# Order of the expert loads: the rows of the next group ahead of a group's weights, and two weight blocks instead of four ahead of the first gather

## The chip, the cores and the metric

One core of a Trainium2 chip. The metric is device microseconds (us) of one execution, median over runs; lower is better. Engines are TensorE (PE, with PEld for its weight loads), VectorE (DVE), ScalarE (ACT), GpSimd (POOL) and SyncE (SP), each of which takes its instructions in order; a wait on a semaphore holds back everything behind it on that engine.

## The reference

Three stages. First a gated linear attention over 4 batches, 8 heads, 768 positions and head width 48, with a complex decay:

```python
for t in range(S):
    new_re = ar * S_re - ai * S_im
    new_im = ar * S_im + ai * S_re
    S_re, S_im = (new_re + kv, new_im)
    y[:, :, t] = np.einsum('bhd,bhde->bhe', q[:, :, t], S_re)
```

Then a mixture of experts with one expert for each token (3072 tokens of width 384, 8 experts of inner width 1024), and last a dense gated layer of inner width 1536:

```python
e_idx = np.argmax(x @ w_gate + modality_bias[modality_id], axis=1)
for e in range(E):
    mask = e_idx == e
    h = np.maximum(x[mask] @ w1[e], 0.0)
    out[mask] = gate_w[mask, None] * (h @ w2[e])
...
g = x @ w_gate
return (silu(g) * (x @ w_val)) @ w_out
```

## The kernel before

The attention runs in chunks of 128 positions and ends with all 24 tiles of 128 rows scaled and stored to `x_scratch`. The router's result is turned into a sorted order of the tokens (`sorted_id`) and, for each group of 384 sorted rows, the number of its expert (`tab` row 0) and the row at which the group begins (`tab` row 1). There are 8 groups' worth of rows and at most 15 groups; here the expert stage runs 9 groups and loads weights for 10.

**The expert stage.** A group t has 8 steps, numbered w = 8t to 8t+7; one step takes 128 of the 1024 inner columns. "Block w" is that step's slice of both expert matrices: two DMAs of 192 KB, issued by SP on lines 724 and 727, into one of RAW = 6 raw buffers. ACT turns the block into the high part of a two-part product (line 1455, `expert_high`), DVE makes the low part (line 1167, `expert_low`, semaphore `s_wl`). Both run AHEAD = 2 steps in front: in step w, ACT does relu(w) and then `expert_high(w+2)`; DVE does `h_low(w)`, then `expert_low(w+2)`, and then, in three steps of each group, a part of the next group's transposed rows (`x_evac`, lines 1160 and 1162). PE does `up(w)` (line 1714, 9 matmuls, waits for `expert_low(w)`), `down(w-1)` (line 1727, 9 matmuls) and in the same three steps a transpose of the next group's rows (`xtr`, line 1701). The three steps are 4, 5, 6 of group 0 and 2, 3, 4 of each later group. In the first step of each group ACT also copies the last group's result out of PSUM (`y_out`, line 1482) when `down` of the last group's step 7 is done.

**The rows.** POOL gathers the first group's rows (three indirect DMAs, line 543, semaphores `s_xf`) straight into the row buffer `xg`. For each later group t it gathers three tiles into a single staging buffer (line 551), waits for them, and stores them in order to `xs_scratch` (line 559, semaphore `s_xs`, 16 more for each group). The gather for group t begins only when the store for group t-1 has landed. From group 3 on it also waits for a step of PE. SP then reads group t's rows from `xs_scratch` with one DMA of 576 KB (`load_rows(t)`, line 738), for which it waits until `s_xs` says that group t is stored (line 732). ACT issues the dense layer's weights in between (line 1465), two of 384 KB when the first rows are gathered, and then one in every third step.

**The order on SP before.** Blocks 0 to 3 go out at once; then SP waits for the first group's three gathers (line 746), and issues blocks 4 to 7, then waits for the store of the first group's rows and for the zeroed tail of `xs_scratch`, and issues `load_rows(1)`. In each later group t, blocks 8t to 8t+3 come first, then `load_rows(t+1)`, then blocks 8t+4 to 8t+7. Block w needs its raw buffer free, which is `s_wl` of at least w-5.

Of the kernel before, what the change touches and what calls it, by code (L numbers as in the profile page):

```python
# [5 lines left out]
def build(nc, q, k, v, a_re, a_im, modality_id, moe_w_gate, modality_bias, w1, w2,  # L6
# [20 lines left out]
    FC = FE // P  # L27
# [21 lines left out]
    MG = NG + NE - 1  # L49
    RAW = 6  # L50
    SLOTS = 4
    AHEAD = 2
# [17 lines left out]
    with ctx:  # L70
# [3 lines left out]
        def sem(name):  # L74
            return ctx.enter_context(nc.semaphore(name))
# [226 lines left out]
        s_zero = sem("xs_zeroed")  # L302
        s_xf = [sem(f"first_rows{i}_gathered") for i in range(TG)]
        s_xs0 = sem("first_rows_stored")
# [39 lines left out]

        X_AT = (2, 3, 4)
        X_AT_FIRST = (4, 5, 6)

        ROWS_FIRST = 4

        PRODUCTS = ((0, 1), (1, 0), (0, 0))  # L350

# [5 lines left out]
        def first_steps(t):  # L357
            return range(t * FC, (t + 1) * FC)
# [19 lines left out]
        def after(eng, x, count):  # L378

            if count > 0:  # L380
                eng.wait_ge(x, count)
# [194 lines left out]
        def _(sp):  # L576
# [141 lines left out]
            def load_weights(w, e):  # L718
                t, f = divmod(w, FC)

                if w >= RAW:
                    sp.wait_ge(s_wl, w - RAW + 1)
                at = w_raw[:, w % RAW]
                sp.dma_start(at[:, 0:KC * P].rearrange("p (k f) -> p k f", k=KC),
                             w1_v[:, ds(e, 1), :, f * P:(f + 1) * P].rearrange("p o k f -> p (o k) f")
                             ).then_inc(s_wr[w % RAW], 16)
                sp.dma_start(at[:, KC * P:PIECE],
                             w2_v[:, ds(e, 1), f, :].rearrange("p o d -> p (o d)")).then_inc(s_wr[w % RAW], 16)

            def load_rows(t):  # L730
                sp.wait_ge(s_tab, 1)
                sp.wait_ge(s_xs, 16 * min(t, NG - 1))
                first = sp.value_load(tab[0:1, 1, t:t + 1], min_val=0, max_val=TOK)

                if t >= 2:
                    sp.wait_ge(s_xTp, KC * (t - 1))
                    after(sp, s_xl[t % 2], 16 * ((t - 1) // 2))
                sp.dma_start(xg[:, t % 2], xs_dram[ds(first, GW), :].rearrange("(i p) d -> p i d", p=P)
                             ).then_inc(s_xl[t % 2], 16)

            def load_group(t):
                e = sp.value_load(tab[0:1, 0, t:t + 1], min_val=0, max_val=NE - 1)
                for w in first_steps(t):
                    if w == ROWS_FIRST:
                        for i in range(TG):
                            sp.wait_ge(s_xf[i], 16)
                    if t > 0 and w % FC == FC // 2 and t + 1 < MG:
                        load_rows(t + 1)
                    load_weights(w, e)
                if t == 0:  # L750
                    sp.wait_ge(s_xs0, 16)
                    sp.wait_ge(s_zero, 16)
                    load_rows(1)

            sp.wait_ge(s_te, 1)
            for t in range(NG + 1):
                load_group(t)
            total = sp.value_load(tab[0:1, 2, 0:1], min_val=NG, max_val=MG)
            more_groups(sp, total, NG + 1, NG, load_group)

            def load_group_yT(g):
# [1043 lines left out]
```

## Time and profile before

| | |
|---|---|
| median of 3 runs | 1021.33 us (1021.08 to 1025.95) |
| the profiled execution | 1021.33 us, span 1019.6 us |
| PE busy | 936.1 us (92%) |
| DVE, ACT, POOL busy | 579.2, 382.2, 175.6 us |
| mean granted TensorE clock | 0.975 |
| expert stage, first to last `up` or `down` | 301.5 to 546.5 us |

The span is the time from the first to the last instruction; 1.73 us lie around it. Times in the rows below count from the start of the span. A DMA's landing is counted from the start of its issue.

### The profile page before, as it was taken

Reading aid. Unit: us, or ns where it says so; the run is one execution under the profiler, and the core shown is the slowest. Engines: PE = TensorE matmul, PEld = TensorE weight load, DVE = VectorE, ACT = ScalarE, POOL = GpSimd, SP = SyncE. Lnnn points to the kernel's source line nnn. Section 1 sums busy time; section 2 is a strip of 40 time slices with the busy share of each in tenths; the row PEclk is TensorE's granted clock in tenths of the full one; section 3 lists DMA queues with packets and bytes.
Section 4 is the critical chain, followed back from the end, with each engine's and each line's share of the span. In section 5 each row is a group of like instructions: output and inputs, shape, how many; then the busy total and the mean of one; then the engine's idle time right before and its main releaser. Section 6 shows DMA issues by size and latency. Waiting matters only on the chain.

```text
span 1019.6 us, 15885 instructions
## 1 busy us (share of the span) xinstructions
PE 936.1 (92%) x6100; PEld 888.9 (87%) x6100; DVE 579.2 (57%) x993; ACT 382.2 (37%) x536; POOL 175.6 (17%) x198
## 2 busy tenths in 40 slices
PE   2688999999959999999999999999999999999994
PEld 0566878888839999999998999999999999999994
DVE  6978777755566666666555445544444444535432
ACT  7987878756434545444342110111101111011110
POOL 6234234531842211100000001010101000010101
PEclk9799999999959999999999999999999999999998
DMA  9998743420368987765454000000101000000000
GB/s 170 156 156 117 112 88 49 63 56 1 126 215 273 331 280 249 248 201 173 153 187 136 1 24 24 24 24 3 45 1 47 1 24 24 24 24 1 24 1 23
DMA packets 211487, 98.83 MB, mean 97 GB/s; under 512 B 150854, under 2 KB 206406, under 8 KB 211403
## 3 DMA queue, kind: packets, MB, share of 16 engines
q1 hardware_dynamic: 197994, 70.19, 30.3%
q0 software_dynamic: 4368, 14.75, 4.2%
q10 hardware_dynamic: 9040, 12.78, 3.9%
q8 instruction: 51, 0.84, 0.3%
q14 instruction: 34, 0.27, 0.1%
HBM read 77.58 MB, written 20.08 MB: 96 GB/s over the span
## 4 chain that ended last, share of the span: by engine, by line
PE 79%; ACT 5%; DVE 5%; issue 5%; DMA 2%; SPq 2%; POOL 1%; ACTq 0%; DVEq 0%; POOLq 0%
PE psum L1759 27%; PE psum L1771 15%; PE psum L1714 9%; PE psum L1727 9%; PE psum L1568 4%; PE psum L1577 3%; PE psum L1558 2%; PE psum L1613 2%; PE psum L1547 2%; PE psum L1594 2%; PE psum L1616 1%; SPq L587 1%; PE psum L1549 1%; PE psum L1701 1%; ACT group_work L1482 1%
## 5 line engine op out<-in xcount | busy, mean ns | idle before, releaser
L1759 PE MATMUL psum<-xT_parts,w_parts 128*128 128x384 f32 x1728 | 316.3, 335 | 2.3 <-DVE xT_parts L1210 2.3
L1759 PEld LDWEIGHTS psum<-xT_parts,w_parts 128*128 128x128 f32 x1728 | 302.3, 189 | 2.6 <-issue 2.6
L1218 DVE TENSOR_TENSOR group_work<-group_work,psum 128x384 f32<-128x384 f32 x96 | 53.2, 554 | 233.1 <-ACT group_work L1526 233.1
L1526 ACT ACTIVATE group_work<-psum 128x384 f32<-128x384 f32 x96 | 47.2, 492 | 355.3 <-PE psum L1759 355.3
L1771 PE MATMUL psum<-w_parts,act_parts 128*128 128x384 f32 x864 | 166.3, 335 | 5.7 <-DVE act_parts L1226 5.7
L1771 PEld LDWEIGHTS psum<-w_parts,act_parts 128*128 128x128 f32 x864 | 150.7, 188 | 8.4 <-DVE act_parts L1226 8.4
L1714 PE MATMUL psum<-xT_parts,expert_parts 128*128 128x384 f32 x648 | 129.3, 344 | 5.4 <-DVE expert_parts L1167 4.5
L1727 PE MATMUL psum<-act_parts,expert_parts 128*128 128x384 f32 x648 | 123.9, 335 | 0.4 <-DVE act_parts L1172 0.4
L1714 PEld LDWEIGHTS psum<-xT_parts,expert_parts 128*128 128x128 f32 x648 | 113.4, 191 | 8.4 <-DVE expert_parts L1167 6.7
L1727 PEld LDWEIGHTS psum<-act_parts,expert_parts 128*128 128x128 f32 x648 | 112.9, 188 | 1.1 <-DVE act_parts L1172 0.8
L569 POOL DMA_INDIRECT out<-group_work,sorted_id x24 | 23.6, 981 | 462.3 <-ACT group_work L1532 457.4
L1167 DVE TENSOR_TENSOR expert_parts<-group_work,expert_parts 128x768 fp32r<-128x768 f32 x74 | 70.9, 958 | 33.0 <-ACT expert_parts L1455 32.2
L1476 ACT ACTIVATE act_parts<-psum 128x384 fp32r<-128x384 f32 x72 | 35.3, 490 | 125.3 <-PE psum L1714 125.3
L1172 DVE SCALAR_TENSOR_TENSOR act_parts<-psum,act_parts 128x384 fp32r<-128x384 f32 x72 | 40.1, 557 | 57.9 <-ACT act_parts L1476 57.9
L1455 ACT ACTIVATE expert_parts<-group_work 128x768 fp32r<-128x768 f32 x74 | 62.2, 841 | 10.8 <-DMA group_work<-in_w 5.9
L1315 ACT ACTIVATE arena<-psum 128x1024 f32<-128x1024 f32 x48 | 49.2, 1024 | 37.3 <-PE psum L1568 37.3
L867 DVE TENSOR_TENSOR arena<-psum,causal 128x512 f32<-128x512 f32 x48 | 33.1, 690 | 46.7 <-PE psum L1577 46.4
L1568 PE MATMUL psum<-ident,arena 128*128 128x128 f32 x384 | 54.0, 285 | 5.7 <-DVE arena L861 4.1
L1568 PEld LDWEIGHTS psum<-ident,arena 128*128 128x128 f32 x384 | 42.7, 144 | 15.2 <-issue 10.4
L1226 DVE TENSOR_TENSOR act_parts<-group_work,act_parts 128x384 fp32r<-128x384 f32 x96 | 53.7, 559 | 3.3
L1219 DVE TENSOR_TENSOR group_work<-group_work,psum 128x384 f32<-128x384 f32 x96 | 53.1, 554 | 3.3
L1577 PE MATMUL psum<-arena 128*128 128x128 f32 x384 | 51.9, 279 | 0.0
(192 smaller groups left out, 1041.6 us busy)
## 6 DMA issues: line engine op xcount, KB each, us to landing
group_work<-in_w SPq DMA_DIRECT2D x160, 192.0 KB, 3.5
group_work<-xs_scratch SPq DMA_DIRECT2D x10, 576.0 KB, 4.7
yT_scratch<-group_work ACTq DMA_DIRECT2D x9, 576.0 KB, 4.4
arena<-in_q SPq DMA_DIRECT2D x24, 192.0 KB, 4.0
arena<-in_k SPq DMA_DIRECT2D x24, 192.0 KB, 4.2
arena<-in_v SPq DMA_DIRECT2D x24, 192.0 KB, 4.4
x_scratch<-x_all SPq DMA_DIRECT2D x24, 192.0 KB, 1.9
xs_scratch<-group_work POOLq DMA_DIRECT2D x8, 576.0 KB, 5.9
```

The costliest lines, as they stand in the source:

```text
L1167: nc.vector.tensor_tensor(low, w_raw[:, w % RAW], high.bitcast(F32), ALU.subtract).then_inc(s_wl, 1)
L1218: link(nc.vector.tensor_tensor(sig[:, w % 2, :], sig[:, w % 2, :], psum[:, w % 2, 0:GW], ALU.mult))
L1219: link(nc.vector.tensor_tensor(sig[:, w % 2, :], sig[:, w % 2, :], psum[:, 2 + w % 2, 0:GW], ALU.mult))
L1226: nc.vector.tensor_tensor(low, sig[:, w % 2], high.bitcast(F32), ALU.subtract).then_inc(s_act, 1)
L1315: nc.scalar.activation(qkT[:, u % 3], psum[:, 2:4, :], ACT.Copy).then_inc(c_tev, 1)
L1455: nc.scalar.activation(we_p[:, w % SLOTS, 0], w_raw[:, w % RAW], ACT.Copy).then_inc(s_wh, 1)
L1568: last = nc.tensor.transpose(psum[:, 2 + j, hh * P:(hh + 1) * P], qk_nat[:, n % 3, j, HG * g + hh, :], ident[:])
L1577: last = nc.tensor.matmul(psum[:, 4 + u % 2, at], qkT[:, u % 3, 1, at], qkT[:, u % 3, 0, at], start=True, stop=True)
L1714: last = nc.tensor.matmul(psum[:, w % 2, 0:GW], we_p[:, w % SLOTS, i, k * P:(k + 1) * P], x_p[:, j, t % 2, k, :], start=(k == n == 0), sto ...
L1727: last = nc.tensor.matmul(psum[:, 4 + k, 0:GW], we_p[:, w % SLOTS, i, at:at + P], act_p[:, j, w % 2], start=(f == n == 0), stop=(f == FC - ...
L1759: last = nc.tensor.matmul(psum[:, b, 0:GW], wt[:, i, k, f * P:(f + 1) * P], x_p[:, j, g % 2, k, :], start=(k == n == 0), stop=(k == KC - 1 ...
L1771: last = nc.tensor.matmul(psum[:, 4 + i, 0:DM], act_p[:, a, w % 2, i * P:(i + 1) * P], w_o_p[:, c, f, :], start=(f == n == 0), stop=(f == ...
```

## The change

The constant ROWS_FIRST goes away. SP now waits for the first group's gathers in front of block 2 instead of block 4. It issues `load_rows(1)`, with its waits, in front of block 6 instead of behind block 7. For each later group t, `load_rows(t+1)`, with its wait for the store of group t+1, stands in front of block 8t instead of block 8t+4. No instruction is added or removed on any engine, and no buffer changes.

```diff
-        ROWS_FIRST = 4
-
...
             def load_group(t):
                 e = sp.value_load(tab[0:1, 0, t:t + 1], min_val=0, max_val=NE - 1)
+                if t > 0 and t + 1 < MG:
+                    load_rows(t + 1)
                 for w in first_steps(t):
-                    if w == ROWS_FIRST:
+                    if w == AHEAD:
                         for i in range(TG):
                             sp.wait_ge(s_xf[i], 16)
-                    if t > 0 and w % FC == FC // 2 and t + 1 < MG:
-                        load_rows(t + 1)
+                    if w == RAW:
+                        sp.wait_ge(s_xs0, 16)
+                        sp.wait_ge(s_zero, 16)
+                        load_rows(1)
                     load_weights(w, e)
-                if t == 0:
-                    sp.wait_ge(s_xs0, 16)
-                    sp.wait_ge(s_zero, 16)
-                    load_rows(1)
```

## Rows read from the trace of the kernel before

**Rows 1.** The page: the chain that ended last, shares of the span by engine.
```profile
PE 79%; ACT 5%; DVE 5%; issue 5%; DMA 2%; SPq 2%; POOL 1%; ACTq 0%; DVEq 0%; POOLq 0%
```
**Rows 2.** The chain that ended last, from 300 to 337: start, us, what.
```profile
300.34 6.65 DMA group_work<-x_scratch,sorted_id
307.28 6.54 DMA xs_scratch<-group_work
314.63 4.37 DMA group_work<-xs_scratch
319.05 0.55 PE psum L1701 x3
...
322.75 0.33 PE psum L1701 x3
...
329.66 1.56 PE psum L1714 x9
331.22 1.57 PE psum L1727 x9
...
334.70 0.86 ACT expert_parts L1455
335.57 0.97 DVE expert_parts L1167
336.59 1.83 PE psum L1714 x9
```
**Rows 3.** SP's timeline: issues of blocks 2, 4, 8, of rows 2, of block 12.
```profile
290.91 0.40 SPq L724 DMA_DIRECT2D group_work<-in_w  x1
...
299.86 0.38 SPq L724 DMA_DIRECT2D group_work<-in_w  x1
...
315.78 0.39 SPq L724 DMA_DIRECT2D group_work<-in_w  x1
...
329.95 0.38 SPq L738 DMA_DIRECT2D group_work<-xs_scratch  x1
...
331.07 0.50 SPq L727 DMA_DIRECT2D group_work<-in_w  x1
```
**Rows 4.** SP's waits over the whole span: us in total, times, longest.
```profile
SPq L732 <- DMA xs_scratch<-group_work: 17.5, 3, 8.3
```
**Rows 5.** POOL's timeline: gathers and a store, idle time before them in brackets.
```profile
293.42 1.25 POOL L543 DMA_INDIRECT group_work<-x_scratch,sorted_id  x1 [3.06 <-DVE sorted_id L1152]
...
297.84 0.95 POOL L551 DMA_INDIRECT group_work<-x_scratch,sorted_id  x1 [0.30 <-issue]
...
324.08 0.80 POOL L559 DMA_DIRECT2D xs_scratch<-group_work  x1 [6.43 <-DMA group_work<-x_scratch,sorted_id]
...
329.43 0.98 POOL L551 DMA_INDIRECT group_work<-x_scratch,sorted_id  x1 [4.55 <-DMA xs_scratch<-group_work]
```
**Rows 6.** L727, block 4's second DMA, issued at 300.43: its landing.
```profile
DMA to landing us min/median/max: 6.4/6.4/6.4
```
**Rows 7.** L727, block 12's second DMA, issued at 331.07: its landing.
```profile
DMA to landing us min/median/max: 6.6/6.6/6.6
```
**Rows 8.** L559, all seven stores of sorted rows: their landing.
```profile
DMA to landing us min/median/max: 4.6/5.2/7.2
```
**Rows 9.** ACT and DVE timeline: parts of block 2, then ACT's part of block 8.
```profile
305.28 0.84 ACT L1455 ACTIVATE expert_parts<-group_work 128x768 fp32r<-128x768 f32 x1
...
306.15 0.96 DVE L1167 TENSOR_TENSOR expert_parts<-group_work,expert_parts 128x768 fp32r<-128x768 f32 x1 [0.18 <-ACT expert_parts L1455]
...
325.06 0.84 ACT L1455 ACTIVATE expert_parts<-group_work 128x768 fp32r<-128x768 f32 x1
```
**Rows 10.** Windows of 1 us: busy PE, PEld, DVE, ACT, POOL, clock, DMA share, GB/s.
```profile
547.00:548.00 1.00, 0.00 (x0) 0.00 (x0) 0.47 (x2) 0.62 (x1) 0.00 (x0) 1.00 0.61 171
...
549.00:550.00 1.00, 1.00 (x4) 1.00 (x5) 0.96 (x3) 0.00 (x0) 0.00 (x0) 0.50 1.02 361
...
552.00:553.00 1.00, 1.00 (x7) 1.00 (x7) 0.00 (x0) 0.48 (x1) 0.00 (x0) 1.00 0.00 0
```

## The prediction, made before the changed kernel ran

> **What bounds the kernel now.** I read the page first. Its chain that ended last is PE for 79% of the span, and waits for a DMA make up 2% [rows 1]. So the kernel is bound by TensorE, and an order of loads can only matter where PE has run out of weights or of rows. I then followed that chain in order of time through the start of the expert stage, since only there does it leave PE for transfers [rows 2]. The reader is to see this in it: the gathers for group 1 (until 306.99), the store of its sorted rows (307.28 until 313.82) and the read of those rows (314.63 until 319.00) stand one behind the other, and PE's first transpose of group 1 starts on that read's landing, at 319.05. From there on the chain is up and down, 1.56 us each, with one short detour over ACT and DVE at the group's first steps (334.70 to 336.59). SP's own timeline tells what was issued when [rows 3], SP's waits show that line 732, the wait for the stored rows, held the queue three times, 8.3 us at most [rows 4], and POOL's timeline shows when each sorted group was stored [rows 5]. The last view is that of the clock beside a short pause of PE [rows 10].
>
> The point to keep: line 732 costs nothing in the kernel before, although SP stands there for 8.3 us, because the blocks that PE needs meanwhile were issued ahead of it. Blocks 8 to 11 went out from 315.78 on [rows 3], and SP then waited for group 2's rows until 329.95. The change puts this same wait ahead of block 8.
>
> **Part 1: blocks 2 and 3 behind the first gathers.** Before, they are issued from 290.91 on [rows 3] and are on the DMA engines while POOL issues the first gathers. The first gather's issue lasts 1.25 us, one issued later into a quieter stretch 0.95 us [rows 5], so 0.3 us each for about two of them, and perhaps 0.1 us of the last landing: I take 0.7 us earlier for the landing of the last first gather. Bounds: 0, if the longer issue has another cause, and 0.9 if all three are 0.3 us shorter. Everything behind it starts that much earlier: PE's first transposes, the dense loads, SP's next issues.
>
> What it costs: block 2 now has the place that block 4 had, issued at 299.86, second half at 300.43, which landed after 6.4 us [rows 3, 6], so at 306.8; ACT took block 2 at 305.28 [rows 9]. Block 2 is thus 1.5 us late for ACT. Its low part on DVE would end at 308.7 in the old times instead of 307.1, and PE takes up(2) at about 308.5, behind down(0). The cover is 1.3 us, so some 0.3 us are lost. Block 3 behind it is wanted a step (3.1 us) later and has the cover. Both fall together with PE's wait for group 1's rows, which stands anyway until they land, so the 0.3 us vanishes there. Part 1 alone: 0.7 us won (0 to 0.9).
>
> **Part 2: rows 1 ahead of blocks 6 and 7.** The bytes in flight between 300 and 314 don't change: four blocks, 2 to 5 in place of 4 to 7. The store of group 1 still ends at 313.8 less 0.7, so rows 1 are issued and land as before, less 0.7. Block 6 now follows them. It had been in its buffer long before. Issued at about 314.4 and 315.0 (0.7 us earlier than the old times, and 0.5 to 1.1 us behind the rows), it lands after 6.4 to 6.6 us, if the two blocks' second halves that were issued beside the same kind of traffic are a guide [rows 6, 7], at about 321.5. ACT's high part takes 0.84, DVE's low part 0.96 [rows 9]. In DVE's queue the first part of group 1's transposed rows stands behind that low part, and PE's second transpose waits for it; it ran at 322.75 before [rows 2]. Now it runs at 321.5 + 0.84 + 0.96 + 1.1 (two DVE passes over the rows) = 324.4, against 322.05 with the 0.7 taken off: 2.4 us of waiting (0 if block 6 lands in 4 us). This counts only if block 8 is in time, because a later wait for a fixed landing swallows it.
>
> **Part 3: rows 2 ahead of block 8.** Here the terms of the sum are. Queued on SP behind the wait for group 2's store are blocks 8 to 13. On ACT, relu(7), two dense weight copies and block 9 stand behind block 8; on DVE, the last part of group 1's rows and h_low(7); PE then stands in front of up(8), since nothing ahead of it in its own queue is left after down(6).
>
> - The store of group 2 ended 0.3 us before POOL's next gather at 329.43, so at 329.1 [rows 5]. It moves by the 0.7 of part 1, and by up to 0.5 because blocks 10 and 11 are not in flight beside it (it took 5.1, the shortest of all seven 4.6 [rows 8]). I take 328.0; bounds 327.0 and 329.3.
> - SP's wait to its issue of rows 2: 329.95 - 329.1 = 0.8. Rows 2 go out at 328.8.
> - Block 8 is next. Block 12 had exactly this place before: rows 2, then block 12, beside the same gathers of group 3. Its second half was issued at 331.07 and landed after 6.6 us, at 337.7, which is 7.7 us after rows 2 were issued at 329.95 [rows 3, 7]. So block 8 lands at 336.5. Bounds: 6.4 and 8.7 us instead of 7.7.
> - High and low part: 0.86 + 0.97 with the gaps between, 1.9 in all [rows 2]. up(8) starts at 338.4. Before, it started at 329.66 [rows 2]. That is 8.7 us later, and PE stands idle for about 7 of them, from down(6)'s end at some 331.4.
> - The clock. After a pause of 2 us between the expert and the dense stage PE's granted clock fell to 0.50 (1.2 GHz) as work began again and was back at 1.00 three us later, [rows 10]. Three to three and a half us at half rate are 1.6 us lost. A longer pause should do at least this once: 1.6, bounds 0 and 3.2.
>
> What is late next: nothing for long. h_low(7) and the copy of group 0's result come late by the same amount and their own chain from down(7)'s end to up(10), 332.8 to 336.6 before, keeps its 3.8 us [rows 2]. Blocks 9 to 13 follow block 8 at once, since their buffers are free. Rows 3, 4 and on stand ahead of blocks 16, 24 and on, and are reached 4 blocks earlier than before. Group 3's store was issued at 339.5 and was the slowest of the seven, 7.2 us [rows 8]; it ended at 346.7, so block 16 would go out at some 347 and land at 355, and ACT wants it in step 14, 13 us after up(10), which is past 360. From group 4 on POOL's store is finished some 7 us before SP gets there. These moves are hidden, and would cost whole microseconds in each group if that distance were gone. Nothing waits later that could give the time back: PE is the bound to the end, and a late group stays late.
>
> **Sum:** 8.7 + 1.6 = 10.3 us, made against the profiled execution's own 1021.33 us, which is the median of the runs as well: 1031.6 us.
>
> One rule of the Trainium skill bears on the 328.0. Row: group 2's gathers, on POOL's queue, landed at 323.8, 0.3 us before the store's issue at 324.08 [rows 5], while SP's blocks 8 to 11 were queued from 315.78 on [rows 3]. The page DMA: Bandwidth & Descriptors, section Queues, rings and completion order, says that each DMA engine takes turns between the queues with work, a packet at a time. By that, blocks 10 and 11, last in SP's own queue, take nothing from the gathers while 8 and 9 are undrained, and the store begins where I have it; if all queued bytes shared equally, two blocks fewer of about eight would bring the gathers in some 1.5 us earlier, and the sum would be 8.8 us, 1030.1. No row before separates the two.
>
> The same page, section Rules for kernel authors, speaks against the change: issue a DMA early, wait for it late. Block 8 goes out 13 us later than before. By the rule the time is worse.
>
> **Rivals.**
>
> *A. Faster or level: less traffic brings the sorted rows in time.* The sort is a chain of gather, store, gather, store. Part 1 frees it of two blocks. For block 8 to be ready at 329.66 it must land at 327.7, rows 2 must be issued by 320.0, and group 2's store must have landed by 319.2, ten us earlier than it did. For it: in quiet stretches a store takes 4.6 [rows 8] instead of 6.5 [rows 2], and a group of gathers three issues of 0.95 with 0.3 between and some 3 us to land, about 5.6, instead of the 9.2 from 297.84 to 306.99 [rows 2, 5]; two of each from 297.8 give some 318.5. Against it: after 300 the same number of blocks and the same two dense loads are in flight as before, so the stretch isn't quiet; only 0.7 us is won at its head. If it came out so, only part 1 is left: 1020.6, or 1023.0 with block 6's wait. The point from which it decides is group 2's store landing before 320. For a gain of over 5 us no row offers a source.
>
> *B. Slower, but half as much.* Block 8 overtakes part of the rows' traffic, or the dense load that now is held back on ACT leaves room, and the clock stays up: 327.0 + 0.8 + 6.4 + 1.9 = 336.1, 6.4 us late, 1027.8.
>
> *C. Slower by more.* No gain from part 1 (329.3), block 8 lands after 8.7 us since six blocks are now issued in one burst, and two stretches at half clock: 329.3 + 0.8 + 8.7 + 1.9 - 329.7 = 11.0, plus 3.2, is 14.2: 1035.5.
>
> **Chances.** The sum within 2 us, 0.50; B and what lies between, 0.22; C and beyond, 0.14; A 0.10, and in it 0.03 for a gain over 0.5%; 0.04 for anything else that leaves it within 0.5%. 0.5% is 5.1 us, about what a measurement of this kernel can tell from no change. So faster 0.03, same 0.11, slower 0.86. The range that holds 8 in 10 leaves out A and the far end of C: 1027.0 to 1035.0.
>
> **What would show it.** In the profile after: the last first gather lands near 299.0; block 2's high part starts near 306 and up(2) is within 0.5 us of where it was; rows 1 land near 318.3; PE's second transpose of group 1 comes about 2 us late; group 2's store lands near 328, rows 2 are issued near 328.8, block 8 near 329.4, and PE stands idle from about 331 to 338 in front of line 1714, released by DVE's line 1167; the granted clock falls to 0.5 there; from step 10 on the distance to the kernel before stays near 10 us. SP's waits name line 732 for more than 17.5 us, and line 724 for less. The prediction is wrong if group 2's rows are stored before 320, if block 8 lands in less than 5 us, or if rows 3 and later hold SP long enough for a second wait of PE.

## The result, and the profile after

| | before | after |
|---|---|---|
| median of 7 runs | 1021.51 us (1021.08 to 1025.95) | 1031.44 us (1028.12 to 1036.35) |
| profiled execution, and its span | 1021.33, 1019.6 us | 1028.27, 1026.5 us |
| up(0) starts | 301.5 | 301.5 |
| up(8) starts | 329.66 | 334.48 |
| up(10) starts | 336.59 | 344.37 |
| first matmul of the dense layer | 548.8 | 556.3 |

The changed kernel is slower: ratio 1.0096, interval 1.0067 to 1.0125. Its times spread over 8 us, and the trace is of one of the shortest executions; a second trace of the same kernel (`e8_after_again`, below) is of a longer one.

Line numbers after are two lower: `up` is line 1712, `down` 1725, the wait for stored rows 730. In the lines of the experiments they shift by one to three with each edit.

The page after, first part and the chain that ended last. PE is busy for 2.9 us more than before and its weight loads for 1.4, the other engines are within 1 us of where they were, and the share of DMA in the chain is the same 2% as in [rows 1]: shares of the whole span don't show the loss.

```profile
PE 939.0 (91%) x6100; PEld 890.3 (87%) x6100; DVE 578.6 (56%) x993; ACT 382.3 (37%) x536; POOL 174.6 (17%) x198
...
PE 78%; ACT 6%; issue 5%; DVE 5%; DMA 2%; SPq 2%; POOL 1%; ACTq 0%; DVEq 0%; POOLq 0%
```

The chain that ended last in the changed kernel, in order of time, for the stretch that answers to [rows 2] (start, us, what):

```profile
300.40 5.80 DMA group_work<-x_scratch,sorted_id
...
306.49 6.81 DMA xs_scratch<-group_work
...
322.33 3.77 DMA xs_scratch<-group_work
...
326.89 0.38 SPq L736
...
327.93 4.64 DMA group_work<-in_w
332.59 0.85 ACT expert_parts L1453
333.47 0.97 DVE expert_parts L1165
...
334.48 3.25 PE psum L1712 x9
337.73 2.87 PE psum L1725 x9
340.63 1.14 ACT group_work L1480
...
343.35 0.97 DVE expert_parts L1165
...
344.37 1.86 PE psum L1712 x9
```

Before, this chain was on PE from 319.05 on, but for the short detour over ACT and DVE [rows 2]. Now it stays with the sort for the whole way: gathers of group 1, its store, the gathers of group 2, its store (322.33, 3.77 us), SP's issue of rows 2 and then of block 8, block 8's landing, its high and low part, and only then PE, at 334.48. PE's first two products behind the pause take 3.25 and 2.87 us instead of 1.56.

SP's timeline after, the lines that answer to [rows 3] (block 2; rows 1 and block 6; rows 2 and block 8). Block 6's first half is issued 0.6 us behind rows 1, block 8's 0.6 us behind rows 2, and between 316.33 and 326.89 SP issues nothing:

```profile
300.23 0.40 SPq L722 DMA_DIRECT2D group_work<-in_w  x1
...
314.11 0.39 SPq L736 DMA_DIRECT2D group_work<-xs_scratch  x1
314.69 0.38 SPq L722 DMA_DIRECT2D group_work<-in_w  x1
...
316.33 0.35 SPq L725 DMA_DIRECT2D group_work<-in_w  x1
326.89 0.38 SPq L736 DMA_DIRECT2D group_work<-xs_scratch  x1
327.45 0.37 SPq L722 DMA_DIRECT2D group_work<-in_w  x1
```

SP's waits over the whole span, for [rows 4]. The wait for stored rows grew by 1.8 us only, from 17.5. What changed is what stands behind it:

```profile
SPq L730 <- DMA xs_scratch<-group_work: 19.3, 3, 8.9
```

The timeline of all engines after, lines that answer to [rows 5, 9]: the three first gathers; ACT's part of block 2 and PE's up(2); the store of group 2's rows and the gather behind it; ACT's part of block 8 and PE's up(8). The bracket is the idle time before and what ended it:

```profile
293.51 1.53 POOL L541 DMA_INDIRECT group_work<-x_scratch,sorted_id  x1 [3.06 <-DVE sorted_id L1150]
295.34 1.00 POOL L541 DMA_INDIRECT group_work<-x_scratch,sorted_id  x1 [0.30 <-issue]
296.65 0.94 POOL L541 DMA_INDIRECT group_work<-x_scratch,sorted_id  x1 [0.30 <-issue]
...
308.51 0.84 ACT L1453 ACTIVATE expert_parts<-group_work 128x768 fp32r<-128x768 f32 x1 [3.10 <-DMA group_work<-in_w]
...
310.40 1.83 PE L1712 MATMUL psum<-xT_parts,expert_parts 128*128 128x384 f32 x9 [1.67 <-DVE expert_parts L1165]
...
322.33 0.80 POOL L557 DMA_DIRECT2D xs_scratch<-group_work  x1 [5.20 <-DMA group_work<-x_scratch,sorted_id]
326.37 0.99 POOL L549 DMA_INDIRECT group_work<-x_scratch,sorted_id  x1 [3.24 <-DMA xs_scratch<-group_work]
...
332.59 0.84 ACT L1453 ACTIVATE expert_parts<-group_work 128x768 fp32r<-128x768 f32 x1 [6.02 <-DMA group_work<-in_w]
334.48 3.25 PE L1712 MATMUL psum<-xT_parts,expert_parts 128*128 128x384 f32 x9 [3.42 <-DVE expert_parts L1165]
```

The first gather's issue takes 1.53 us, longer than the 1.25 before, though only blocks 0 and 1 are issued ahead of it. Block 2 ends ACT's idle time at 308.51, 1.7 us later than forecast, and costs PE 1.67 us. PE then stands idle for 3.42 us in front of up(8).

The clock, in windows of 1 us (columns as in [rows 10]). It falls during the pause and stays at 0.50 (1.2 GHz) for about 6.8 us, twice as long as before at the start of the dense layer:

```profile
332.00:333.00 1.00, 0.00 (x0) 0.00 (x0) 0.00 (x0) 0.41 (x1) 0.00 (x0) 1.00 1.03 312
...
334.00:335.00 1.00, 0.52 (x2) 0.52 (x3) 0.97 (x3) 0.55 (x2) 0.00 (x0) 0.50 1.13 326
...
339.00:340.00 1.00, 1.00 (x5) 1.00 (x4) 0.00 (x0) 0.00 (x0) 0.00 (x0) 0.50 1.17 368
...
341.00:342.00 1.00, 1.00 (x7) 0.98 (x6) 0.00 (x0) 0.76 (x1) 0.00 (x0) 1.00 1.02 406
```

### The profile page after: what moved, and what is told of

The parts are those of the page before. It is cut to its first block, busy times and chain, and to the rows that moved or that the text cites. A ratio compares the mean times of both kernels' runs of the same rounds, so it can differ in the third digit from the quotient of the medians.

```text
span 1026.5 us, 15885 instructions
## 1 busy us (share of the span) xinstructions
PE 939.0 (91%) x6100; PEld 890.3 (87%) x6100; DVE 578.6 (56%) x993; ACT 382.3 (37%) x536; POOL 174.6 (17%) x198
## 4 chain that ended last, share of the span: by engine, by line
PE 78%; ACT 6%; issue 5%; DVE 5%; DMA 2%; SPq 2%; POOL 1%; ACTq 0%; DVEq 0%; POOLq 0%
PE psum L1757 27%; PE psum L1769 15%; PE psum L1712 9%; PE psum L1725 9%; PE psum L1566 4%; PE psum L1575 3%; PE psum L1556 2%; PE psum L1611 2%; PE psum L1545 2%; PE psum L1592 2%; PE psum L1614 1%; PE psum L1547 1%; SPq L585 1%; DMA xs_scratch<-group_work 1%; ACT group_work L1480 1%
```

## The experiments

Each was timed against the kernel before on the same chip. Diffs are against the kernel that the text names.

### e1_parts12: rows of the later groups back at block 8t+4

Against the changed kernel:

```diff
-                if t > 0 and t + 1 < MG:
-                    load_rows(t + 1)
                 for w in first_steps(t):
...
+                    if t > 0 and w % FC == FC // 2 and t + 1 < MG:
+                        load_rows(t + 1)
                     load_weights(w, e)
```

> Parts 1 and 2 of the change stay (wait for the first gathers in front of block 2, rows 1 in front of block 6); the rows of each later group are back in front of block 8t+4. My theory, that the whole loss is block 8 standing behind the store of group 2: block 8 goes out early, and what is left is between 0 and 2.5 us over the kernel before, 1021 to 1024 us. Rival, that the late blocks 2 and 6 carry a part of the loss: 1025 us or more.

Measured: 1023.16 us against 1022.04, ratio 1.0013 (1.0002 to 1.0024). Parts 1 and 2 together cost about 1 us (0.2 to 2.4 by the interval) and win nothing. The loss is in part 3.

### e2_rows2_ahead: the kernel before, with rows 2 alone in front of block 8

Against the kernel before:

```diff
-                    if t > 0 and w % FC == FC // 2 and t + 1 < MG:
+                    if t > 0 and w == (FC if t == 1 else t * FC + FC // 2) and t + 1 < MG:
                         load_rows(t + 1)
```

> The kernel before with one move only: rows 2 in front of block 8 instead of block 12. Parts 1 and 2 and all later groups as before. My theory: the whole loss returns, 1029 to 1033 us. Rival, that the loss needs parts 1 and 2 as well or is spread over the later groups: 1022 to 1026 us.

Measured: 1033.63 us against 1022.04, ratio 1.0118 (1.0102 to 1.0134). One DMA moved past four blocks on one queue brings back the whole loss; the time is 0.6 us over the range expected. Its timeline shows the same pause as the changed kernel's:

```profile
334.93 3.25 PE L1714 MATMUL psum<-xT_parts,expert_parts 128*128 128x384 f32 x9 [4.97 <-DVE expert_parts L1167]
```

### e4_rows2_back: the changed kernel, with rows 2 alone back in front of block 12

Against the changed kernel:

```diff
-                if t > 0 and t + 1 < MG:
+                if t > 1 and t + 1 < MG:
                     load_rows(t + 1)
...
+                    if w == FC + FC // 2:
+                        load_rows(2)
                     load_weights(w, e)
```

> The changed kernel with one move undone: rows 2 are back in front of block 12; parts 1 and 2 and rows 3 and on stay ahead of their group's blocks. My theory: within 1 us of the kernel with parts 1 and 2 alone, 1021 to 1024 us. Rival, rows ahead of blocks 16, 24 and on hold PE up in the later groups: 2 us or more over that kernel.

Measured: 1022.37 us against 1022.04, ratio 1.0002 (0.9992 to 1.0011). All other moves of the change together cost and win nothing that can be measured. Parts 1 and 2 are among them, so the 1 us of e1 isn't seen here; the two intervals overlap. So the later groups, where rows go ahead as well, are hidden, as forecast: there line 730 of the changed kernel never waits after 345 us.

The trace is of its longest execution, 1029.15 us. In it the first gather is issued at 299.10 and up(0) starts at 307.04, each some 5.6 us later than before, so most of what it has over the median was lost ahead of everything that the change touches. It also has the wait that the prediction expected from part 2, PE's second transpose of group 1 held up by block 6:

```profile
329.99 0.52 PE L1701 MATMUL psum<-ident,group_work 128*128 128x128 f32 x3 [2.05 <-DVE xT_parts L1162]
```

### e3_fill: work for PE during the pause

Against the changed kernel, in `up`:

```diff
+                if w == FC:
+                    for _ in range(28):
+                        nc.tensor.matmul(psum[:, 2, 0:P], ident[:], ident[:], start=True, stop=True)
                 pe.wait_ge(s_wl, w + 1)
```

> The changed kernel with 28 matmuls of 128 columns on the identity put in front of up(8), into a PSUM bank that nothing reads any more; they take about 3.3 us and end before or about when block 8 is ready (334.5 in the trace after). If the clock's fall after PE's pause is a term of its own, the two products behind the pause take 1.56 us each instead of 3.25 and 2.87, and the time is 2 to 5 us under the changed kernel's, 1026 to 1029 us. If the pause alone counts: the same as the changed kernel, 1031 us, or up to 1 us more.

Measured: 1029.07 us (1028.62 to 1032.66) against 1022.04, ratio 1.0080 (1.0064 to 1.0095). The changed kernel's two measurements are 1.0096 and, below, 1.0109, so the fill takes 1.6 to 2.9 thousandths off, 1.6 to 3 us. The intervals overlap, so the times alone don't show a gain. The traces are clearer. Each f32 product on the identity is two matmuls in the trace, so the fill took 6.4 us instead of the 3.3 expected and filled the pause whole:

```profile
334.39 0.84 ACT L1453 ACTIVATE expert_parts<-group_work 128x768 fp32r<-128x768 f32 x1 [8.27 <-DMA group_work<-in_w]
...
330.44 6.41 PE L1706 MATMUL psum<-ident 128*128 128x128 f32 x56
336.61 1.83 PE L1715 MATMUL psum<-xT_parts,expert_parts 128*128 128x384 f32 x9
```

up(8) starts at 336.61, 2.1 us later than in the changed kernel's trace, of which 1.8 are block 8 itself (ACT takes it at 334.39, there at 332.59). It takes 1.83 instead of 3.25, and up(10) starts at 344.29, as early as there (344.37). The second trace of the changed kernel (e8, below) has block 8 as late as this one, at 334.84, and no fill: its up(10) starts at 346.08, 1.8 us later than here. The granted clock stays at 1.00 throughout. From up(8) to up(10) it is 7.7 us, against 9.9 in the changed kernel and 6.9 before. So the fall of the clock is a term of its own, of some 2 us.

### e6_rows2_at9 and e7_rows2_at10: rows 2 in front of block 9, or of block 10

The same edit as in e4, with `w == 9` and `w == 10` in place of `w == FC + FC // 2`.

> The changed kernel with rows 2 in front of block 9 instead of block 8. Rows 2 are issued at 327 to 330 and block 9 lands 5.7 to 7.7 us later, 333 to 337; before, ACT took block 9 at 328.5 and PE ran up(9) at 332.6. So up(9) is 2.4 to 6.5 us late, some of it made up by the stall that the copy of group 0's result makes anyway behind it: 1024 to 1028 us, clearly between the changed kernel and the one with rows 2 in front of block 12. Rival, that any wait of SP ahead of the blocks costs the same whatever block stands behind it: 1031 us.

> The changed kernel with rows 2 in front of block 10. Block 10 lands at 333 to 337; ACT took it at 334.7 before, behind the copy of group 0's result. So 0 to 2.5 us late: 1022 to 1024.5 us. Rival as for block 9: 1031 us.

| rows 2 in front of block | median | before beside it | ratio (interval) |
|---|---|---|---|
| 8 (the change, again) | 1032.97 | 1022.38 | 1.0109 (1.0088 to 1.0130) |
| 9 | 1027.82 | 1022.38 | 1.0047 (1.0034 to 1.0060) |
| 10 | 1024.34 | 1022.38 | 1.0017 (1.0004 to 1.0030) |
| 12 (e4) | 1022.37 | 1022.04 | 1.0002 (0.9992 to 1.0011) |

The price depends on which block stands behind the wait: one block further is worth 5 us, the next 3.5, and after two more it is gone. Both e6 and e7 lie in the range expected for them. A step of PE is 3.1 us. The first block is worth more than that, and the traces offer the clock for it: 6.8 us at half in both traces of the changed kernel, 3.4 in e6's, none in e7's. The length of the pause doesn't explain this by itself, since e6's is no shorter than the 3.42 us of the changed kernel's first trace:

```profile
342.16 2.96 PE L1714 MATMUL psum<-xT_parts,expert_parts 128*128 128x384 f32 x9 [3.51 <-DVE expert_parts L1167]
```

(This trace, too, is of an execution whose up(0) starts late, at 307.01.) In e7's timeline ACT waits for block 10 only 1.90 us, having copied group 0's result in the meantime, and PE waits 1.83 in front of up(10):

```profile
337.08 0.84 ACT L1455 ACTIVATE expert_parts<-group_work 128x768 fp32r<-128x768 f32 x1 [1.90 <-DMA group_work<-in_w]
...
338.97 1.86 PE L1714 MATMUL psum<-xT_parts,expert_parts 128*128 128x384 f32 x9 [1.83 <-DVE expert_parts L1167]
```

### e8_after_again: a second trace of the changed kernel

The changed kernel, unchanged.

> The changed kernel once more, for a second trace and more times, since its times spread over 8 us (1028.1 to 1036.4) and its trace is of one of the shortest. My theory of the spread: the landing of block 8 (332.6 in the first trace) and the number of stretches at half clock behind the pause differ between executions. So a second trace with a time 2 us or more over 1028.3 shows up(8) starting later than 334.5 or a longer stretch at 0.50 behind it, or both, together by as much as the difference. Rival: the difference lies elsewhere, in the attention or the dense stage. Median 1030 to 1033 us.

Measured: 1032.97 us (1030.65 to 1037.18) against 1022.38, ratio 1.0109 (1.0088 to 1.0130). The trace has a span of 1029.7 us, 3.2 over the first. Its timeline, with the gather behind group 2's store, the issue of rows 2, ACT's part of block 8, up(8) and up(10):

```profile
328.20 0.99 POOL L549 DMA_INDIRECT group_work<-x_scratch,sorted_id  x1 [4.12 <-DMA xs_scratch<-group_work]
...
328.72 0.37 SPq L736 DMA_DIRECT2D group_work<-xs_scratch  x1
...
334.84 0.84 ACT L1453 ACTIVATE expert_parts<-group_work 128x768 fp32r<-128x768 f32 x1 [8.89 <-DMA group_work<-in_w]
...
336.73 3.25 PE L1712 MATMUL psum<-xT_parts,expert_parts 128*128 128x384 f32 x9 [6.29 <-DVE expert_parts L1165]
...
346.08 1.85 PE L1712 MATMUL psum<-xT_parts,expert_parts 128*128 128x384 f32 x9 [0.62 <-DVE expert_parts L1165]
```

Group 2's store ends 1.8 us later than in the first trace, PE's pause is 6.29 us instead of 3.42, and up(8) starts 2.25 us later. At up(10) the two are 1.7 us apart. So rather more than half of the 3.2 us is where the theory has it, in the landing of block 8; the length of the stretch at half clock is the same. The rest lies behind: 0.2 by the start of the dense layer (558.2 and 556.3), 1.3 within and after it (its last gate product starts at 1013.0 and 1009.8). This is the rival's place, and the clock again. PE pauses there in both traces; in the first its clock stays up, in the second it falls. First the changed kernel's first trace, then the second:

```profile
556.30 7.13 PE L1757 MATMUL psum<-xT_parts,w_parts 128*128 128x384 f32 x36 [2.21 <-DVE xT_parts L1208]
561.00:562.00 1.00, 1.00 (x8) 1.00 (x7) 0.79 (x2) 0.14 (x1) 0.00 (x0) 1.00 0.56 69
```

```profile
558.21 8.67 PE L1757 MATMUL psum<-xT_parts,w_parts 128*128 128x384 f32 x36 [2.40 <-DVE xT_parts L1208]
561.00:562.00 1.00, 1.00 (x5) 1.00 (x4) 0.00 (x0) 0.42 (x1) 0.00 (x0) 0.50 0.00 0
```

The same 36 matmuls take 1.5 us longer. Of the twelve traces of this case, eight have this fall, that of the kernel before among them [rows 10], and four don't (the first of the changed kernel, e1, e2 and e3).

### e5_six_ahead: six blocks beside the first gathers

Against the kernel before:

```diff
-        ROWS_FIRST = 4
+        ROWS_FIRST = 6
```

> The kernel before with the wait for the first gathers in front of block 6: six blocks instead of four (the changed kernel: two) are in flight beside the first gathers. If weight traffic slows the gathers, as part 1 of my prediction had it, the last of the first gathers lands 0.5 to 1.5 us later than in the kernel before (299.7 in its trace) and the time is 1022 to 1023.5 us. The traces so far speak for the rival, that the longer issue of the first two gathers is not from that traffic: landing within 0.3 us of before, time 1021 to 1022 us.

Measured: 1023.29 us against 1022.38, ratio 1.0006 (0.9991 to 1.0022), the same within the measurement and in the range expected. Its trace goes against the rival: the last of the first gathers, issued at 296.62, lands after 5.3 us, not 3.1 us, and PE's first product starts at 303.2 instead of 301.5. So traffic does delay a gather's landing, when there is enough of it. But four blocks, as before, are hardly enough. The first gather lands after 3.9 to 4.2 us with four and after 3.3 to 3.5 with two, but the last, which PE waits for, after 3.1 and 3.0; and from the first gather's issue to the landing of the last it is 6.3 us in the kernel before, 6.2 in the changed kernel and in e1, and 5.9 in e8.

### e9_copy_later and e10_after_copy_later: the copy of a group's result behind the block

Against the kernel before, and against the changed kernel, in ACT's `group`:

```diff
-                    if w % FC == 0 and 0 < t < NG:
-                        y_out(t - 1)
                     if w + AHEAD < MG * FC:
                         expert_high(w + AHEAD)
+                    if w % FC == 0 and 0 < t < NG:
+                        y_out(t - 1)
```

> The kernel before, with ACT's copy of the last group's result moved behind its part of block 8t+2 in the first step of each group. Nothing of the change is in it. In the trace before, PE waits 0.6 to 0.76 us in front of up(8t+2) at seven group boundaries, released by DVE's line 1167, which waited for ACT, which did the copy first; the page puts 4.5 us on that wait. With the order turned, ACT does its part of the block while it would wait for down(7). My theory: those waits go, 4 to 5 us less, 1017 to 1018.5 us. Rival: the copy comes 0.85 us later, PE's down(8) waits for it, and nothing is won: 1021.5 to 1022.5 us.

> The changed kernel with the same move. If the loss of the change is block 8's late landing and the clock behind it, and not this copy, it stays whole: 1026 to 1029 us, again 9 to 11 us over the kernel before with the same move. Rival: a part of the loss is the copy's chain behind the late down(7), and goes with it: less than 8 us over.

Measured: on the kernel before, 1016.43 us against 1022.40, ratio 0.9929 (0.9912 to 0.9947); on the changed kernel, 1024.87 us, ratio 1.0023 (1.0008 to 1.0039). The first is faster than both kernels of this case. Both times lie below the ranges expected, since the move wins 6 us and not 4 to 5. PE's waits for DVE's line 1167 at the group boundaries are gone. The group of `up` in e9, whose 5.4 us of idle time before it had 4.5 of them:

```profile
L1714 PE MATMUL psum<-xT_parts,expert_parts 128*128 128x384 f32 x648 | 128.5, 343 | 0.9 <-issue 0.9
```

These account for 4.5 of the 6 us; what makes the rest was not looked for. The change on top of the move costs 8.4 us by the medians and 9.6 by the ratios, where without it the medians differ by 9.9 and 10.6. The 9.6 lies in the theory's 9 to 11 us, the 8.4 between that and the rival's less than 8. So the loss stays for the most part with the copy out of the way; whether 1 us of it is the copy's chain, the measurement doesn't tell.

## Why the prediction was right, point by point

The forecast of 1031.6 us in the sum and slower as the sign held: 1031.44, and the cause is the one it named. That the two lie 0.2 us apart is luck. The changed kernel's times spread over 8 us, and two terms of the sum were off in opposite directions: block 8's lateness was taken 3.9 us too high against the first trace and 1.6 against the second, the clock's price 1.4 and 0.8 too low. A small term, part 1, brought nothing.

- **Rows 2 ahead of block 8 is the whole loss.** Shown: e2 makes it alone, e4 takes it away alone.
- **The store of group 2, taken at 328.0.** It landed at 326.1 in the first trace after, at 327.9 in the second. The store took 3.77 and 4.65 us against 5.1 before, and the lower bound of 327.0, made with the shortest of seven stores (4.6), was not low enough. SP issues nothing there for 10 us. That alone doesn't make the store short: in e3, where SP issues nothing either, it took 5.2.
- **Block 8 lands 7.7 us after the issue of rows 2.** 5.7 us in the first trace, 6.1 in the second; both are below the bound of 6.4. Block 12 was the right place to read from, but not with the right neighbours: before, ACT's dense load was issued at 328.85, a microsecond ahead of it, and in the changed kernel that load is held back on ACT behind block 8. In e7, where it is issued at 330.09 beside rows 2, block 10 lands after 7.5 us; in e6, where it is held back, block 9 lands after 6.0, and in e2 and e3 block 8 after 6.0 and 5.9. That fits, but no run moved the dense load alone. Rival B had named this.
- **up(8) 8.7 us late.** 4.8 in the first trace, 7.1 in the second. PE idled for 3.4 and 6.3 us, not for 7.
- **The clock, 1.6 us.** Mis-sized: from up(8) to up(10) it takes 9.9 and 9.35 us against 6.93 before, 3.0 and 2.4 more. The clock was at half for about 6.8 us instead of 3.4, and two products of nine matmuls fell into it. e3 shows some 2 us of it to be the clock.
- **The two together.** 4.8 + 3.0 = 7.8 us in the first trace and 7.1 + 2.4 = 9.5 in the second, where the spans are 6.9 and 10.1 us over that of before. The sum had 10.3. The kernel before has the fall of the clock at the start of the dense layer in its trace, the first trace after doesn't, the second does; that is some 1.5 us between the spans which differs from execution to execution of one kernel.
- **Part 1, 0.7 us won.** This step was wrong. The long issues of the first two gathers were put down to the weight traffic; they are about as long with half of it (1.53 and 1.00 us after, 1.25 and 1.30 in e1, 1.25 and 0.95 in e8; before 1.25 and 1.32). The last first gather lands at 299.7 as before, not at 299.0, and the time shows no gain.
- **Block 2, 0.3 us lost, and then hidden.** It landed 7.7 us after its second half's issue, not 6.4, and up(2) started at 310.40 instead of 308.45. PE reached group 1's transposes 0.8 us late for that reason, and rows 1 were there, so the lateness did not vanish in the wait for them. In e1's trace up(10) starts 0.95 us later than before, which may be the 1 us of e1; e4 doesn't show it in the time.
- **Block 6.** It landed 5.6 us after its second half's issue, and PE waited 0.46 us for the transposed rows, not 2.4. In other executions it is more, 2.05 us in e4's trace, so the term was not empty. As forecast, the pause in front of up(8) swallows it.
- **The signs.** The clock, the idle time in front of line 1714 and the wait on line 732 came as named. Three small ones did not: the first gathers and up(2), as above, and SP's wait for free raw buffers on line 724, which was to shrink and grew from 115.5 to 122.6 us (line 722 after). Of the three that were to show the prediction wrong, "block 8 lands in less than 5 us" is not clear: counted from rows 2, as in the sum, it is 5.7 and 6.1, but from the issue of its own second half it is 4.6 and 5.1.
- **The later groups are hidden, and nothing gives the time back.** Shown by e4, and by the distance: 7.8 us at up(10), 7.5 at the first matmul of the dense layer.
- **Rival A**, that less traffic brings the rows in time, needed group 2's store to land by 319.2. It came 7 us after that. With the Trainium skill's rule on turns between queues (DMA: Bandwidth & Descriptors, Queues, rings and completion order) the prediction had let the gathers of group 2 land no earlier, with the other reading 1.5 us earlier. They were issued from 313.57 and landed at 322.0, 8.5 us later, where before it was 9.7 from 314.09. That is 1.2 us less, but it is no evidence for either reading: in the second trace the same gathers took 9.0 us, and in e1, where blocks 6 to 11 are all out beside them, 8.5.

## What to carry to other kernels

When a load is moved ahead on a queue, ask what its wait stands in front of, not how long it waits: here the wait grew by 1.8 us and the kernel by 10, because the blocks that had covered it now stood behind it. Price such a move by the slack of the first item behind the wait; each place further back gave back 5 and 3.5 us, and two more places the last 2, where a step of the bound engine is 3.1. The same question pays on any engine that works in order: turning two instructions on ACT, so that it works on the next block while it would wait for the last result, was worth 6 us, where no order of the loads that was tried here won anything.

## What the runs showed of the hardware that was not expected

- TensorE's clock stayed at 0.50 for about 6.8 us around the end of pauses of 3.42 (changed kernel), 4.97 (e2) and 6.29 us (e8), but for about 3.4 us around the end of one of 3.51 us (e6). At the start of the dense layer, behind pauses of 2.12 to 2.47 us, it fell for about 3.4 us in some executions and not in others, and made 1.5 us of difference between two executions of one kernel. Pauses of 1.83 (e7) and 2.05 us (e4) in the expert stage left it at 1.00.
- Keeping PE busy with products that nobody reads kept the clock at 1.00 (e3). From up(8) to up(10) it then took 7.7 us instead of 9.9.
- The issue of the first indirect gather took 1.25 to 1.53 us in every trace looked at, with two, four or six blocks issued ahead, and of a later one in a quiet stretch 0.95 us. The number of weight blocks doesn't explain it; what does was not tried.
- Weight traffic beside the first gathers isn't paid in proportion: with two blocks issued ahead the last of them landed after 3.0 us, with four after 3.1, with six after 5.3. The first landed after 3.3 to 3.5 us with two and 3.9 to 4.2 with four.
